# One block of programs for the dense stage and the experts, and a result turned on VectorE

## The reference

```python
def _moe_ref(x, w_in, w_out):                 # dense: 384 -> 2048 -> 384, 3072 tokens
    h = x @ w_in
    sp = np.where(h > 20.0, h, np.log1p(np.exp(np.minimum(h, 20.0))))
    return (h * np.tanh(sp)) @ w_out

def _moe2_ref(x, w_gate, w1, w2):             # experts: N, D, E, F = 3072, 384, 8, 1024
    logits = x @ w_gate
    P = np.exp(logits - logits.max())
    for _ in range(8):                        # Sinkhorn rounds
        P /= P.sum(1, keepdims=True) + 1e-09
        P /= P.sum(0, keepdims=True) + 1e-09
        P *= N / E
    out = np.zeros((N, D))
    for e in range(E):
        out += P[:, e:e + 1] * (np.maximum(x @ w1[e], 0.0) @ w2[e])
    return out
```

## Time and profile before

| | us |
|---|---|
| median of 3 runs (lowest, highest) | 2551.49 (2548.61, 2552.88) |
| the profiled execution, its own time | 2551.59 |
| its span, first to last instruction | 2549.7 |
| attention, until 527 | 527 |
| dense, until 934 | 407 |
| gate and fold, until 957 | 23 |
| experts and result, until the end | 592.7 |
| PE busy | 2480.8 (97% of the span) |
| mean granted TensorE clock | 0.972 of full |

### The profile page before, as it was taken

One profiled execution on the slowest core, in us unless ns is written; L12 is line 12 of the kernel. 1 busy time (PEld: TensorE's weight loads), 2 busy tenths in 40 slices (PEclk: granted clock), 3 DMA queues, 4 the chain that ended last, 5 costly groups with the idle time before them and its releaser, 6 DMA issues.

```text
span 2549.7 us, 40196 instructions
## 1 busy us (share of the span) xinstructions
PE 2480.8 (97%) x15472; PEld 2093.3 (82%) x15472; DVE 1280.6 (50%) x2409; ACT 886.0 (35%) x1922; POOL 429.4 (17%) x350
## 2 busy tenths in 40 slices
PE   6989999989999989999999999999999999999999
PEld 5889888878888868888888888888888888888887
DVE  4766657668777754434333333333333333333333
ACT  4767567746666641111111111111111111111112
POOL 6674556400000010100000000000000000000000
PEclk8998789989999999999999999999999999999999
DMA  1110010020000010101101101101101101011001
GB/s 60 44 44 22 23 43 29 10 75 25 0 0 0 0 51 1 43 9 46 42 13 47 42 13 47 42 13 44 40 17 42 37 22 42 11 48 42 17 25 67
DMA packets 27092, 78.81 MB, mean 31 GB/s; under 512 B 2936, under 2 KB 6456, under 8 KB 25016
## 3 DMA queue, kind: packets, MB, share of 16 engines
q1 hardware_dynamic: 22472, 62.94, 7.2%
q10 hardware_dynamic: 4464, 13.50, 1.5%
HBM read 71.61 MB, written 4.82 MB: 30 GB/s over the span
## 4 chain that ended last, share of the span: by engine, by line
PE 63%; DMA 0%; DVE 0%; issue 0%; SPq 0%; ACT 0%
PE ex_h L51 31%; PE ex_y L51 31%; PE ex_logits L51 1%; DMA ex_fold<-fold 0%; DVE ex_term L1088 0%; DVE ex_acc L1102 0%; ACT ex_stage L1029 0%; SPq L914 0%; SPq L913 0%; ACT ex_gate L990 0%; DVE ex_gate L1041 0%
## 5 line engine op out<-in xcount | busy, mean ns | idle before, releaser
L1124 DVE SCALAR_TENSOR_TENSOR ex_r_lo<-ex_h,ex_r_hi 128x512 fp32r<-128x512 f32 x384 | 264.5, 689 | 944.2 <-ACT ex_r_hi L1014 944.2
L1014 ACT ACTIVATE ex_r_hi<-ex_h 128x512 fp32r<-128x512 f32 x384 | 229.8, 598 | 1274.4 <-PE ex_h L51 1274.4
L51 PE MATMUL ex_h<-x_hi,ex_w_hi 128*128 128x512 f32 x1152 | 451.0, 392 | 0.0
L51 PE MATMUL ex_h<-x_hi,ex_w_lo 128*128 128x512 f32 x1152 | 449.2, 390 | 0.0
L51 PE MATMUL ex_h<-x_lo,ex_w_hi 128*128 128x512 f32 x1152 | 449.2, 390 | 0.0
L51 PE MATMUL ex_y<-ex_r_hi,ex_w_hi 128*128 128x512 f32 x1152 | 448.4, 389 | 0.0
L51 PE MATMUL ex_y<-ex_r_hi,ex_w_lo 128*128 128x512 f32 x1152 | 448.2, 389 | 0.0
L51 PE MATMUL ex_y<-ex_r_lo,ex_w_hi 128*128 128x512 f32 x1152 | 448.1, 389 | 0.0
L967 POOL TENSOR_TENSOR ex_w_lo<-ex_stage,ex_w_hi 128x512 fp32r<-128x512 f32 x96 | 123.2, 1286 | 1717.2 <-ACT ex_w_hi L1001 1681.6
L51 PEld LDWEIGHTS ex_h<-x_hi,ex_w_lo 128*128 128x128 f32 x1152 | 216.8, 188 | 45.5
L51 PEld LDWEIGHTS ex_h<-x_hi,ex_w_hi 128*128 128x128 f32 x1152 | 216.8, 188 | 45.1 <-issue 0.5
(11 more groups left out here) (135 smaller groups left out, 3395.7 us busy)
## 6 DMA issues: line engine op xcount, KB each, us to landing
ex_stage<-w_exp SPq DMA_DIRECT2D x15, 1536.0 KB, 6.4
ex_pb<-p_rows SPq DMA_DIRECT2D x90, 256.0 KB, 3.2
at_qT<-q_t ACTq DMA_DIRECT2D x10, 512.0 KB, 4.1
at_v_in<-v ACTq DMA_DIRECT2D x11, 384.0 KB, 3.0
at_k_in<-k ACTq DMA_DIRECT2D x10, 384.0 KB, 4.7
out<-ex_stage SPq DMA_DIRECT2D x5, 768.0 KB, 3.7
de_stage<-w_in SPq DMA_DIRECT2D x8, 384.0 KB, 3.2
de_stage<-w_out SPq DMA_DIRECT2D x8, 384.0 KB, 3.2
```

Source lines behind the costliest of these rows:

```text
L51: return nc.tensor.matmul(out, lhsT, rhs, start=start, stop=stop)
L1014: nc.scalar.activation(r[0][:, j, :], h_bank[j][:], ACT.Relu).then_inc(hi_ready, 1)
L1124: nc.vector.scalar_tensor_tensor(out=r[1][:, j, :], in0=h_bank[j][:], scalar=0.0, in1=r[0][:, j, :].bitcast(F32), op0=ALU.max, op1=ALU.sub ...
```

## The change

- The dense stage and the experts share one Block. `dense_programs` makes the dense stage's programs for the five engines, and each engine runs the dense one and goes on with the experts without meeting the others. Both stages share the banks `h_bank` and `y_bank`. Their SBUF tiles lie at fixed places in one area, so that tiles of the experts reuse places that the dense stage has finished reading.
- The last dense block is written out, and inside its chunks ACT and DVE split the gate's weights, SP loads the first expert's weights (after 8 chunks' `h`), ACT casts them in chunks 10 to 15, and POOL subtracts after 8 chunks' `down`.
- The fold matmuls go. The 16 rows of gate logits are written to DRAM (192 KB) and read back with 24 tokens to a partition (2048 runs of 96 B); DVE adds hi and lo. The probabilities are `[P, E, NT]` now, and go to `p_rows` by one DMA (1024 runs of 96 B) without a turn on PE.
- The Sinkhorn slots start two slots (one step) later and run into the first expert's second half.
- Blocks 0 to 4 of the result are turned by DVE in 32 by 32 pieces (`turn_back`, three 128x512 instructions a block), and the stores put the pieces in place: 12 DMAs a block, each of 32 partitions and 512 runs of 128 B. Block 5 is turned by PE's transpose, per chunk m of the last `down`s, copied by ACT and DVE in turns, and stored as before.

```diff
+Dense = namedtuple("Dense", "sp pool act dve pe h_read w2_read h_taken x_split")
+def dense_programs(nc, s, at, h_bank, y_bank, w_in, w_out, x_hi, x_lo, MC, N, F):
 ...
         with eng.Fori(1, NB - 1) as tb:
             for f in range(FC):
                 step(tb, f, True)
+        for f in range(FC):
+            step(NB - 1, f, True)
 ...
+            if isinstance(tb, int) and tb == NB - 1:
+                extra(f)
 ...
+    def h_read(f):
+        return h_done, (NB - 1) * FC + f
+    def w2_read(f):
+        return down_done, (NB - 1) * FC + f
+    return Dense(sp_program, pool_program, act_program, dve_program, pe_program,
+                 h_read, w2_read, (hn_ready, NB * FC), lambda tb: (xlo_ready, (tb + 1) * MC))
 ...
+    SH = 2
+        g_bank = [l_bank] + h_bank + y_bank
+        turn = stage[:].rearrange("p (b m t) -> p b m t", b=2, m=MC)
         @block.sync
         def _(sp):
+            dense.sp(sp)
             sp.dma_start(gate_in[:], w_gate).then_inc(gate_loaded, 16)
+            sp.wait_ge(*dense.h_read(DF // 2))
+            sp.dma_start(stage[:], w_exp[0, 0]).then_inc(staged0, 16)
+            sp.wait_ge(gated_ready, NB)
+            sp.dma_start(lg_rows, logitsT).then_inc(lg_stored, 16)
+            sp.wait_ge(lg_stored, 16)
+            sp.dma_start(lg[:], lg_rows.rearrange("e (p c) -> p e c", p=P)).then_inc(lg_loaded, 16)
             sp.dma_start(ident[:], masks[:, 0, :]).then_inc(ident_loaded, 16)
             def store(b):
-                sp.wait_ge(turned_out, (b + 1) * TC)
-                sp.dma_start(out[b * TB:(b + 1) * TB, :].rearrange("(t p) d -> p t d", p=P),
-                             out_tile[:, b % 2]).then_inc(stored[b % 2], 16)
+                for m in range(MC):
+                    sp.wait_ge(turned, b * MC + m + 1)
+                    for q in range(P // 32):
+                        to = out[b * TB:(b + 1) * TB, m * P + q * 32:m * P + (q + 1) * 32]
+                        sp.dma_start(to.rearrange("(k i) j -> i k j", i=32),
+                                     turn[q * 32:(q + 1) * 32, b % 2, m, :].rearrange("i (k j) -> i k j", j=32)).then_inc(
+                            stored[b % 2], 16)
             def step(e, g, tb):
 ...
-                    sp.wait_ge(probT_ready, 1)
-                    for i in range(2):
-                        sp.dma_start(p_rows[:, i * HT * P:(i + 1) * HT * P].rearrange("e (c t) -> c e t", c=HT),
-                                     probT[:, i, :]).then_inc(rows_stored, 16)
-                    sp.wait_ge(rows_stored, 32)
+                    sp.wait_ge(cnorm_ready, ROUNDS)
+                    sp.dma_start(p_rows.rearrange("e (p c) -> p e c", p=P), prob[:]).then_inc(rows_stored, 16)
+                    sp.wait_ge(rows_stored, 16)
                 load_pb(e, g, tb)
-                if last_group(e, g) and tb >= 3:
-                    store(tb - 3)
+                if last_group(e, g) and tb >= 2:
+                    store(tb - 2)
         @block.gpsimd
+            dense.pool(pool)
+            pool.wait_ge(*dense.w2_read(DF // 2))
             for i in range(PIECES):
                 split(0, 0, i)
         @block.scalar
+            def prepare(f):
+                if f == 0:
+                    act.wait_ge(gate_loaded, 16)
+                    nc.scalar.copy(gate[:, :, 0, :], gate_in[:].rearrange("p (m e) -> p m e", m=MC)).then_inc(ghi_ready, 1)
+                if f >= DF - PIECES:
+                    split(0, 0, f - DF + PIECES)
+            dense.act(act, prepare)
         @block.vector
+            def turn_back(b, m):
+                if b == 0 and m == 0:
+                    dve.wait_ge(wlo_ready, 2 * E * PIECES)
+                if b >= 2:
+                    dve.wait_ge(stored[b % 2], (b // 2) * 16 * MC * (P // 32))
+                dve.wait_ge(acc_ready, ((2 * E - 1) * NB + b) * MC + m + 1)
+                nc.vector.transpose(turn[:, b % 2, m, :], acc[:, m, b * TB:(b + 1) * TB]).then_inc(turned, 1)
+            def sinkhorn(slot):
+                if slot == 0:
+                    dve.wait_ge(lg_loaded, 16)
+                    nc.vector.tensor_tensor(logits[:], lg[:, 0:E, :], lg[:, E:2 * E, :], ALU.add).then_inc(logits_ready, 1)
+                    dve.wait_ge(logits_ready, 1)
+                    nc.vector.tensor_reduce(top[:, 0:1], logits[:].rearrange("p e c -> p (e c)"), AX.X, ALU.max).then_inc(top_ready, 1)
 ...
-                    if first(e) and g == 0 and j % 2 == 0:
-                        sinkhorn(2 * tb + j // 2)
+                    if first(e) and j % 2 == 0:
+                        sinkhorn(2 * (g * NB + tb) + j // 2 - SH)
 ...
                         for m in range(MC):
                             add(*previous(e, g, tb), m)
+                        if last_group(e, g) and tb > 0:
+                            for m in range(MC):
+                                turn_back(tb - 1, m)
         @block.tensor
+            dense.pe(pe)
             pe.wait_ge(glo_ready, 1)
+            pe.wait_ge(*dense.h_taken)
             for tb in range(NB):
+                pe.wait_ge(*dense.x_split(tb))
 ...
-            for t in range(NT):
-                if t % TC == 0:
-                    pe.wait_ge(gated_ready, t // TC + 1)
-                last = mm(nc, l_bank[:, t * E:(t + 1) * E], logitsT[:, t * P:(t + 1) * P], fold_t[:])
-            last.then_inc(logits_done, 1)
 ...
-                    if last_group(e, g) and tb >= 2:
-                        turn(tb - 2, j)
             def tail():
+                for m in range(MC):
+                    down(E - 1, 1, NB - 1, FC - 2, [m])
+                    down(E - 1, 1, NB - 1, FC - 1, [m])
+                pe.wait_ge(ident_loaded, 16)
+                for m in range(MC):
+                    pe.wait_ge(acc_ready, 2 * E * NB * MC - MC + m + 1)
+                    for t in range(TC):
+                        at = slice((NB - 1) * TB + t * P, (NB - 1) * TB + (t + 1) * P)
+                        last = nc.tensor.transpose(h_bank[t][:, m * P:(m + 1) * P], acc[:, m, at], ident[:])
+                        if m == MC - 1:
+                            last.then_inc(last_turned, 1)
```

More of the change, by code:

```diff
@@ L12 @@
+from collections import namedtuple
 from contextlib import ExitStack
@@ L622, in dense_phase @@
     assert FC % R == 0 and FC % PIECE == 0 and LAG < R
[L624 to L653, removed]
-            for f in range(FC):
[L656 to L694, removed]
-                real, count = past(tb, f, 2)
[L696 to L774, removed]
-                        nc.vector.tensor_tensor(x_lo[:, m, at], y_bank[m][:], x_hi[:, m, at].bitcast(F32),
-                                                ALU.subtract).then_inc(xlo_ready, 1)
-            run(dve, step)
-        @block.tensor
-        def _(pe):
-            def step(tb, f, new):
-                if new:
-                    if isinstance(tb, int):
-                        pe.wait_ge(wlo_ready, pieces.index((0, f // PIECE)) + 1)
-                    real, freed = past(tb, f, R)
-                    if real:
-                        pe.wait_ge(hn_ready, freed)
-                    at = bass.ds(tb * TB, TB)
-                    for m in range(MC):
-                        last = three(nc, h_bank[f % R][:], [w[:, f, m, :] for w in w1],
-                                     [x[:, m, at] for x in (x_hi, x_lo)], start=(m == 0), stop=(m == MC - 1))
-                    last.then_inc(h_done, 1)
-                real, count = past(tb, f, LAG)
-                if real:
-                    fd = (f - LAG) % FC
-                    if isinstance(tb, int) and new:
-                        pe.wait_ge(wlo_ready, pieces.index((1, fd // PIECE)) + 1)
-                    pe.wait_ge(lo_ready, count)
-                    for m in range(MC):
-                        if fd == 0 and not isinstance(tb, int):
-                            pe.wait_ge(xlo_ready, (tb - 1) * MC + m + 1)
-                        last = three(nc, y_bank[m][:], [w[:, fd, m * P:(m + 1) * P] for w in w2],
-                                     [g_hi[fd % R][:], g_lo[fd % R][:]], start=(fd == 0), stop=(fd == FC - 1))
-                        if fd == FC - 1 and m < MC - 1:
-                            last.then_inc(y_done, 1)
-                    last.then_inc(down_done, 1)
-            run(pe, step)
@@ L812, in experts_phase @@
-def experts_phase(nc, w_gate, fold, masks, w_exp, out, x_hi, x_lo, MC, N, E, F):
+    half = FC // 2 * CH * 4
+    w1 = [at(f"w1_{n}", 2 * i * half, [P, FC, MC, P], F32R) for i, n in enumerate(("hi", "lo"))]
+    w2 = [at(f"w2_{n}", (4 + 2 * i) * half, [P, FC, MC * P], F32R) for i, n in enumerate(("hi", "lo"))]
+    small = 8 * half
+    col = 4 * TB
+    stage = [at(f"stage{i}", small + 4 * i * PIECE * CH, [P, PIECE * CH]) for i in range(2)]
+    small += 8 * PIECE * CH
+    en = [at(f"en{i}", small + i * col, [P, TB]) for i in range(2)]
@@ new lines, in run, with past, sp_program @@
+    def run(eng, step):
+        for f in range(FC):
```

(24 more changed lines are left out.)

301 lines of the change are left out of this document (200 added, 101 removed).

## The result

The changed kernel takes 2567.47 us (median of 6 runs, 2559.96 to 2571.96), the kernel before 2552.18 beside it (6 runs): ratio 1.0055, 95% interval 1.0034 to 1.0077. The forecast was 2518. The profiled execution took 2566.9, its span 2565.0.

The account below looks back on a forecast made before the run. The prediction took TensorE's chain of waits to bound the kernel. From 2551.6 us it took gains of 36.2 (seam 18.4, turns 11.5 and 0.4, tail 5.9), added 2.9 for stores, and forecast 2518, range 2512 to 2538.

Parts of the forecast that it names:

- What bounds the kernel now: Opening step, on TensorE: edits pay only through less TensorE work, less idle or slow-clock time at the seam, or shorter tail.
- The seam: Between dense stage and experts: 32.8 us from last dense matmul to first `down` shrink to 14.4, a gain of 18.4.
- what hides the weights: End of the dense stage: load, casts and POOL's six subtractions of 1.29 us finish before the first `h` needs them.
- The turns: Last half of the experts: 16 turns of 0.72 us leave TensorE, 11.5 us gained, plus 0.4 for the probabilities.
- VectorE's transposes: Last half: 0.63 us each on DVE, hidden, since three may take 6.6 us before the `down` waiting for `r_lo`.
- The stores: Result stores in short runs: 30 ns a run and ring, 2.9 us exposed at the end.
- my formula: Exposed store time at the end is 384 d - 8.6 us for price d per run: nothing up to 22 ns.
- rival 2: Stores: every short write costs two passes, 70 ns a run; 60 us exposed, time 2576; chance 0.07.
- The tail: After the last matmuls' start: 9.8 us instead of 15.7, with `acc` ready at 5.7; a gain of 5.9.
- Sinkhorn one step later: First expert: eighth round ends in step 6, probabilities there by 24.6 us, DVE wants them at 25.5; hidden, no cost.
- The rounds keep their rhythm: Sinkhorn in the first expert: rounds run at their old pace, POOL having 1.5 us a step more than fits.
- None of the five: Store backlog 0.13, doubled store price 0.07, transposes bounding DVE 0.04, seam giving back less 0.08; fifth is the forecast itself, 0.68.

Follow-up runs that it names:

- p4: The kernel before with 32 unused bytes behind x, so weights, r and g tiles shift and x stays: 2581.02 us, ratio 1.0127.
- p5: The changed kernel with TensorE's expert loop at a fetch block's head and the gate's two small tiles moved behind the common area: 2523.01 us, ratio 0.9887.
- p13: As p7, with 32 unused bytes ahead of x, so x, weights, r and g all shift together: 2520.29 us, ratio 0.9877.
- p2: The changed kernel with TensorE's expert loop starting at the first instruction of a 256-instruction fetch block: 2553.01 us, ratio 1.0004.
- p8: The kernel before with TensorE's expert loop starting at slot 239 of a fetch block's 256: 2556.56 us, ratio 1.0025.
- p9: The changed kernel with a branch hint for the back edge of TensorE's expert loop, its place left alone: 2555.06 us, ratio 1.0011.
- p7: As p5, with GpSimd subtracting the first expert's weights after the dense stage's last but one down: 2520.87 us, ratio 0.9882.
- p10: As p7, with VectorE's part of the eighth Sinkhorn round moved to the end of its step, behind `r_lo`: 2514.37 us, ratio 0.9855.
- p11: As p7, with the load of the second expert's first weights issued behind the write of the probabilities: 2516.47 us, ratio 0.9857.
- p1: The changed kernel with a 32 B pad ahead of the common area, so weights, r and g start at multiples of 64 B: 2575.58 us, ratio 1.0085.
- p6: As p2, with the common area 96 B further on, its tiles at multiples of 256 B: 2557.0 us, ratio 1.0023.

## Why the prediction was wrong

**The step that failed** is the first one, in "What bounds the kernel now": "an edit pays only in three ways". I took the 1293 us in the middle and the dense stage as given, because no instruction in them changes. Two things changed for them that no line of the diff names: the distance between weights and x in SBUF, and the place of the loop in the instruction stream. They cost 32.1 and 16.4 us, 48.5 of the 49, where the sum had nothing. The balance of the profiled execution, against 2518.3:

| term | us | shown by |
|---|---|---|
| slower pitch, 864 matmuls of `h` dense, 3456 experts; a little in `y` | +32.1 | p4, p5, p13 |
| five pauses at the loop's head | +16.4 | p2, p8, p9 |
| end of the dense stage, GpSimd against VectorE (+5.0), its start and middle (-1.4) | +3.6 | p7 for the 5.0; rows |
| wait at the last Sinkhorn round | +1.4 | p10, p11 |
| seam +0.1, tail +0.8 | +0.9 | rows |
| stores hidden, where 2.9 were forecast | -2.9 | rows |
| attention over sooner in this execution (first dense matmul at 531.65, before 534.22) | -2.6 | varies with the execution: 527.7 to 538.4 in the other traces |

The sum is 2567.2; measured were 2566.9.

**The seam: right.** Last dense matmul, first gate matmul, first `h`, first `down`:

```profile
939.63 0.39 PE L52 MATMUL ex_y<-de_g_hi,de_w_lo 128*128 128x512 f32 x1
939.86 0.40 PE L52 MATMUL ex_logits<-x_hi,ex_gate 128*16 128x512 f32 x1
...
948.12 0.39 PE L52 MATMUL ex_h<-x_hi,ex_w_hi 128*128 128x512 f32 x1
...
954.41 0.39 PE L52 MATMUL ex_y<-ex_r_hi,ex_w_hi 128*128 128x512 f32 x1
```

14.55 us where 14.4 were forecast. But the sentence "what hides the weights" is wrong: POOL's six subtractions were counted as ending in time, not as work beside VectorE. The Trainium skill, GPSIMD Engine Reference, has in the table of its section Specifications that GpSimd shares its SBUF interfaces with VectorE and contends with VectorE's instructions that have two SBUF inputs. The rows agree (1.67 against 0.68, both inputs in SBUF). It would have named this term, though it gives no size for it.

**The turns: right.** Steps of the last half lasted 16.59 at the slower pitch, 16.32 in p5 and after. VectorE's transposes took 0.63 each, the value chosen, and `r_lo` behind them was met:

```profile
2482.75 1.89 DVE L1139 STREAM_TRANSPOSE ex_stage<-ex_acc 128x512 f32<-128x512 f32 x3
```

**The stores: mechanism right, price too high.** Window over most of block 1's stores:

```profile
2484.30:2491.00 6.70, 6.70 (x30) 5.45 (x30) 1.62 (x4) 1.19 (x2) 0.00 (x0) 1.00 0.75 117
```

The 6144 runs of a block took 6.6 to 8.0 us, so 17 to 21 ns a run and ring, where I took 30. At that price my formula exposes nothing, and nothing was exposed: block 4's runs end at 2558.47, the last stores start at 2561.08. The doubled price that rival 2 drew from the Trainium skill's rule on writes under 512 B does not show in these runs.

**The tail: 10.65, forecast 9.8.** `acc` was ready after 5.8, with 5.7 forecast. Behind it the estimate left out that the four last stores are issued one after the other, 1.82 us:

```profile
2560.21 0.66 PE L1250 MATMUL ex_h<-ex_ident,ex_acc 128*128 128x128 f32 x4 [0.69 <-DVE ex_acc L1130]
2560.58 0.86 ACT L1060 COPY ex_out_last<-ex_h 128x384 f32<-128x384 f32 x2 [7.43 <-PE ex_h L1250]
2561.08 1.82 SPq L988 DMA_DIRECT2D out<-ex_out_last  x4
```

**Sinkhorn one step later: wrong by 1.4 (4.6 in p7).** "The rounds keep their rhythm" missed a new neighbour. Before, GpSimd's last sum was over before its last subtraction for the first expert, and so before the next load of weights. One step later it runs beside that load (p11). The slack was thin already: the last round ended at 1053.40, `r_lo` behind it needs 0.7, and the `down` that wants it came at 1053.13 + 2.04 = 1055.17, 1.1 us later.

**Rivals.** None of the five named either cause. Slower was there only through the price of a store, which was refuted.

**With the two placements set right, the forecast holds.** p5 took 2523.0, 5 us above the forecast and inside its range. A part of that is balance: the 2.9 us charged for the stores were not due, and set off some of the three terms that had been left out (GpSimd beside VectorE, the wait at the last Sinkhorn round, the issue of the last stores). p10 took 2514.4, with two of these three removed; that is 1.5% faster than the kernel before. The change itself is worth 1.1%; what hid it was 288 bytes ahead of an area and the address of a loop.

## What to carry to other kernels

When a change moves tiles or code, compare the pitch of untouched matmuls (two starts in the timeline, or nine in the chain) before reading anything else: 0.2334 instead of 0.2267 is 3% on the matmuls that it hits, and no wait shows it. Keep the distance between weights and moving tile at a multiple of 512 B, as the fast kernels here had it, and give a long loop's TensorE program a fixed head or a hint. Price work that is moved beside other work by what the two do to each other, not only by whether it ends in time.

## What the runs showed of the hardware

**Distance of weights and moving tile.** With x 128 B past a multiple of 256: weights at the same offset modulo 2048, `h` 0.2267; 32 B further (p4) 0.2334; 288 (changed) 0.2334; 320 (p1) 0.2333; 384 (p6) 0.2329. At 2.4 GHz 0.2334 - 0.2267 is 16 cycles, as a mean: in the changed kernel most starts of `h` are by turns 0.2317 and 0.2350 apart. With x moved along (p13) 0.2267 again. These are distances of whole tiles. The pieces that single matmuls read start at multiples of 512 B in a weight tile and of 2048 B in x, so all multiples of 512 occur among the fast matmuls. Open: which distances between them are free, and by what mechanism the others cost.

`y` goes from 0.2267 to 0.2274 (changed), 0.2289 (p1) and 0.2293 (p6), though its own tiles keep their distance from their weights. The loss sits right behind `h`: in the experts of the changed kernel the first `y` of a nine takes 0.2325 and the other eight 0.2267; in p1 and p6 the first five take 0.2306 and 0.2315 on average and the last four 0.2267. So it comes from the `h` ahead. Why it reaches further in p1 and p6 is open.

**The loop's head.** With slot 0, or a hint, or the place it had before, no pause; with 17 instructions ahead of a block's end (p8), 1.1 us; in the changed kernel 2.7. The Trainium skill, Runtime: NRT & Kernel Launch, Instruction fetch mechanics, says that instructions are fetched in blocks of 16 KiB, 256 instructions, and that after a taken branch to a target outside the fetched window the engine has to wait for the target's block. The packets agree in size. The rows show another block to be late. In both kernels the first matmul of the body starts in time, so the target's block is there; in p8 the pause begins where the 17 instructions end, and it ends 1.4 us after a packet has landed. Where the head lies in its block in the changed kernel is not on record; that its pause is of the same kind is read from the packets and from p2.

**GpSimd's sum over partitions** ended 6.3 us after the subtraction ahead of it (p11), and 9.5 us after it (p7) beside a load of 1536 KB. The Trainium skill, SBUF — State Buffer, section on the two separate sides, says that DMA and engine accesses to SBUF can't conflict; where these two meet no run here shows.

**GpSimd and VectorE.** A subtraction of GpSimd and a product of VectorE with both inputs in SBUF hold each other up; the one that began later took longer: 1.67 instead of 0.68 for the product, 1.83 instead of 1.29 for the subtraction. In p7 the subtraction stands beside VectorE's `x_lo`, which has one input in PSUM: 0.69 and 1.29 to 1.30.
